# FFT filter and two MLPs on one core: half-height filter loads, a two-part store of the first spectrum, and an earlier first tile

## The chip, the core and the metric

The kernel is one program on one NeuronCore of a Trainium2 chip. Five engines run their own instruction streams and meet at semaphores: TensorE (PE, matmuls; its weight loads are shown as PEld), VectorE (DVE), ScalarE (ACT), GpSimd (POOL) and SyncE (SP), which here issues every DMA. The metric is the device time of one launch in microseconds (us). A median of 3 runs is taken; lower is better.

## The reference

```python
def _attn_ref(x, filt_r, filt_i):            # x: (2, 3008, 256)
    X = np.fft.rfft(x, axis=1)
    Y = X * (filt_r + 1j * filt_i)[None, :, :]
    return np.fft.irfft(Y, n=x.shape[1], axis=1)

def _moe_ref(x, w_gate, w_val, w_out, rms_g):   # 6016 tokens, 256 -> 1536 -> 256
    xn = x / np.sqrt(np.mean(x * x, axis=-1, keepdims=True) + 1e-06) * rms_g
    g = xn @ w_gate
    return ((g * (1.0 / (1.0 + np.exp(-g)))) * (xn @ w_val)) @ w_out

def _moe2_ref(x, w_in, w_out, s, b):            # 256 -> 2048 -> 256
    r = np.maximum(x @ w_in, 0.0)
    return (s * (r * r) + b) @ w_out
```

The three run one after the other, all in float32.

## The kernel before

**Front.** The FFT of length 3008 = 47 x 64 is done by matmuls in 16 chunks q (two batches of 8; a chunk is 32 of the 256 channels). For each chunk: DMA of a slab `x_ring` of 96 rows x 4 KB (`load_x`, ring of 3, so chunk q waits for `step1` of chunk q-3); PE `step1` (L341, the length-47 transform, two halves of 4 matmuls); ACT `u_out` (L533) copies it out; PE `step2` (L352, the length-64 transform); DVE `products` (L736 to L738, six multiplies with the filter, three for each half `dp`); POOL `total` (L913, adds the two product planes, one for each `dp`); PE `step3` (L362, inverse length 64); ACT `w_out_copy` (L539) writes the result into `w_fft[b]`. PE's order is software-pipelined: `step2(q)`, `step3(q-1, 0)`, both halves of `step1(q+1)`, `step3(q-1, 1)`.

The filter comes in 8 tiles `f_n` of 128 partitions x 6 KB (`load_f`); rows 64 to 127 are the same filter rows again. Its imaginary part is multiplied by a table of signs on POOL (`sign`, L906), +conj on the lower half and -conj on the upper one; `products(q)` of the first batch waits for sign q through `f_signed`. POOL does signs 0 and 1 first, and `sign(q+2)` behind the two totals of chunk q.

**Turning the layout.** When a batch's 8 chunks are done (`w_done` at 16, and at 32), two stores of 128 partitions x 12 j x 1 KB, 1.5 MB each, write `w_fft[b]` to a DRAM scratch `by_j`; tiles of 376 tokens are read back by `load_z` (two DMAs of 48 rows x 4 KB for one tile, ring of two, waiting for `step4` of the tile before last). PE `step4` (L373, inverse length 47, one call for each half of the channels) and DVE `copy_y` (L743) make the activations `y`. Of the first batch, tile 0 is worked into chunk 12: `step4(0, 0)` stands between `step2(12)` and `step3(11, 0)`, `step4(0, 1)` behind `step3(11, 1)`. The RMS norm of tile 0 (POOL `squares`, PE `sums` L384/L385, DVE, ACT `root`) follows in chunks 13 and 14.

**The two MLPs.** 16 tiles; in the first MLP each has 12 steps c of 12 + 6 matmuls (`gate_val`, `down`; every float32 product is three matmuls of a high and a low part), in the second 16 steps. While tile t runs, `step4(t+2, ...)` stands behind `down` of c = 5 and c = 7. Weights come from DRAM as float32 and are split into high and low parts by ACT, POOL and DVE between other work: `gate` and `down` during the front, `w_val` (`val_raw`) from chunk 14 on, `w_in2` (`in2_raw`) on POOL during the first MLP. `in2_raw` lies where filter tiles and `w_fft[1]` lay, so its load waits for the stores of batch 1 and the last products.

**SP's order** is the order of the DMA queue: x, tables and filters, with `gate` before x 4 and `down_raw` before x 6, then x 8 to 12, the stores of batch 0 between x 13 and x 14, tiles 0 and 1, `val_raw`, tiles 2 and 3 (each behind its `step4` wait), the stores of batch 1, `in2_raw`, and a loop for the other tiles.

Of the kernel before, what the change touches and what calls it, by code (L numbers as in the profile page):

```python
# [42 lines left out]
TB1, TB2, TB3, TB4 = 96, 120, 376, 504  # L43

# [22 lines left out]
def spectrum_tables():  # L67
# [21 lines left out]
    tab[:, TB1:TB2] = np.concatenate([conj, -conj])  # L89
# [6 lines left out]
def build(nc, by_j, x, filt, tab, step4, w_gate, w_val, w_out, rms_g, w_in2, w_out2, scale2, bias2, out):  # L96
    with ExitStack() as ctx:
# [140 lines left out]
        def _(sp):  # L238
# [90 lines left out]
        def _(pe):  # L329
# [197 lines left out]
        def _(a):  # L527
# [13 lines left out]

            def w1_high(i):
# [52 lines left out]
            w_out_copy(1, 1)  # L595
            for q in range(3, ALL - 1):
# [12 lines left out]
                w_out_copy(q - 1, 1)  # L609
                if 4 <= q < 4 + PIECES1D:  # L610
# [113 lines left out]
        def _(dve):  # L724
            nc.vector.memset(warm[:], 1.0).then_inc(warm_set, 1)
            def products(q, dp):

                dve.wait_ge(s2_mm, q + 1)
                if q < CHUNKS:
                    dve.wait_ge(f_signed, q + 1)  # L730
# [65 lines left out]
            for q in range(ALL):  # L796
                if q == 14:
# [5 lines left out]
                if q == 12:  # L803
                    copy_y(0, 0)
# [5 lines left out]
                if q == 12:  # L810
                    copy_y(0, 1)
# [84 lines left out]
        def _(gp):  # L896
# [118 lines left out]
```

## Time and profile before

| | |
|---|---|
| median of 3 runs | 1269.56 us (1268.67 to 1270.31) |
| the profiled execution | 1270.31 us, its span 1268.5 us |
| PE busy | 1248.8 us (98% of the span), 7268 matmuls |
| DVE, ACT, POOL busy | 685.4, 551.8, 163.7 us |
| mean granted clock of TensorE | 0.993 of full speed |
| DMA | 41.06 MB; 40.54 MB of them on SP's queue |

In slices of 1/40 of the span (31.7 us), the page shows PE at 8 8 8 9 tenths busy and 9 after that, the DMA engines at 9 6 7 3 2 tenths and near 0 later, and the granted clock below full speed in the first two slices. The MLPs fill the time from slice 4 on. A busy PE counts overlapping matmuls once.

### The profile page before, as it was taken

To read this page: it belongs to the slowest core of one execution; us is meant where nothing else is said; L and a number is where in the kernel's file an instruction comes from. 1 tells how busy PE (TensorE), PEld (TensorE's weight loads), DVE (VectorE), ACT (ScalarE), POOL (GpSimd) and SP (SyncE) were. 2 spreads that over 40 slices of the span, in tenths; PEclk is the share of its full clock that TensorE was granted. 3 is DMA by queue.
4 is the path that set the end of the run, shared out by engine and by line. 5 is a ranking of instruction groups with operands and counts; after the bars stand their busy time and mean duration, and the time that the engine had idled before them with its cause. 6 is when DMAs were issued, how large, how long until landed. Compare 5 with 4: busy or idle time off the path is not lost.

```text
span 1268.5 us, 20463 instructions
## 1 busy us (share of the span) xinstructions
PE 1248.8 (98%) x7268; PEld 1216.9 (96%) x7268; DVE 685.4 (54%) x1162; ACT 551.8 (44%) x1108; POOL 163.7 (13%) x165
## 2 busy tenths in 40 slices
PE   8889999999999999999999999999999999999998
PEld 5567999999999999999999999999999999999998
DVE  3566554545454355544554375555556556556555
ACT  2444434324334333433334365455445555455454
POOL 5665210111100111101120030000000000000000
PEclk8899999999999999999999999999999999999999
DMA  9673200000000000000010000000000000000000
GB/s 271 187 237 113 79 14 9 5 13 13 12 12 0 12 12 12 12 0 12 0 66 1 2 1 13 13 13 12 12 12 12 12 12 12 12 12 12 12 4 22
DMA packets 21239, 41.06 MB, mean 32 GB/s; under 512 B 2384, under 2 KB 16336, under 8 KB 20944
## 3 DMA queue, kind: packets, MB, share of 16 engines
q1 hardware_dynamic: 21200, 40.54, 10.5%
q8 instruction: 24, 0.39, 0.1%
q14 instruction: 15, 0.12, 0.0%
HBM read 28.08 MB, written 12.45 MB: 32 GB/s over the span
## 4 chain that ended last, share of the span: by engine, by line
PE 95%; DMA 2%; DVE 1%; POOL 0%; issue 0%; SPq 0%; ACT 0%; POOLq 0%; ACTq 0%
PE bank L388 30%; PE bank L389 30%; PE bank L390 29%; PE bank L373 2%; DMA x_ring<-x 2%; PE bank L341 2%; PE bank L362 1%; PE bank L352 1%; DMA z_ring<-by_j 0%; PE bank L384 0%; PE bank L385 0%; DVE rms L761 0%; DVE prod L738 0%; POOL spec L913 0%; DVE prod L737 0%
## 5 line engine op out<-in xcount | busy, mean ns | idle before, releaser
L783 DVE TENSOR_TENSOR h<-bank,act 128x376 f32<-128x376 f32 x192 | 104.6, 545 | 302.0 <-PE bank L390 293.5
L829 DVE SCALAR_TENSOR_TENSOR h<-act,sc 128x376 f32<-128x376 f32 x256 | 159.5, 623 | 189.6 <-ACT act L649 185.6
L562 ACT ACTIVATE act<-bank 128x376 f32<-128x376 f32 x192 | 92.9, 484 | 365.1 <-PE bank L390 364.9
L649 ACT ACTIVATE act<-bank 128x376 f32<-128x376 f32 x256 | 124.0, 484 | 223.9 <-PE bank L390 223.8
L389 PE MATMUL bank<-h_lo,out_hi 128*128 128x376 f32 x512 | 171.4, 335 | 0.0
L390 PE MATMUL bank<-h_hi,out_lo 128*128 128x376 f32 x512 | 171.4, 335 | 0.0
L388 PE MATMUL bank<-xn_hi,in_hi 128*128 128x376 f32 x512 | 171.1, 334 | 0.2 <-issue 0.2
L388 PE MATMUL bank<-h_hi,out_hi 128*128 128x376 f32 x512 | 171.2, 334 | 0.0
L389 PE MATMUL bank<-xn_lo,in_hi 128*128 128x376 f32 x512 | 171.1, 334 | 0.0
L390 PE MATMUL bank<-xn_hi,in_lo 128*128 128x376 f32 x512 | 170.4, 333 | 0.0
L835 DVE SCALAR_TENSOR_TENSOR h_lo<-h,bi,h_hi 128x376 fp32r<-128x376 f32 x256 | 157.6, 616 | 0.2 <-ACT h_hi L658 0.2
L658 ACT ACTIVATE h_hi<-h,bi 128x376 fp32r<-128x376 f32 x256 | 154.3, 603 | 1.9 <-DVE h L829 1.9
L388 PE MATMUL bank<-xn_hi,gate_hi 128*128 128x376 f32 x384 | 130.9, 341 | 1.2 <-DVE xn_lo L774 1.2
L389 PE MATMUL bank<-xn_lo,val_hi 128*128 128x376 f32 x384 | 128.8, 336 | 0.0
L390 PE MATMUL bank<-h_hi,down_lo 128*128 128x376 f32 x384 | 128.5, 335 | 0.0
L389 PE MATMUL bank<-h_lo,down_hi 128*128 128x376 f32 x384 | 128.5, 335 | 0.0
L388 PE MATMUL bank<-xn_hi,val_hi 128*128 128x376 f32 x384 | 128.3, 334 | 0.0
L389 PE MATMUL bank<-xn_lo,gate_hi 128*128 128x376 f32 x384 | 128.2, 334 | 0.0
L388 PE MATMUL bank<-h_hi,down_hi 128*128 128x376 f32 x384 | 128.2, 334 | 0.0
L390 PE MATMUL bank<-xn_hi,val_lo 128*128 128x376 f32 x384 | 128.2, 334 | 0.0
L390 PE MATMUL bank<-xn_hi,gate_lo 128*128 128x376 f32 x384 | 128.0, 333 | 0.0
L789 DVE TENSOR_TENSOR h_lo<-h,h_hi 128x376 fp32r<-128x376 f32 x192 | 116.7, 608 | 2.6 <-ACT h_hi L569 2.5
(81 smaller groups left out, 2057.2 us busy)
## 6 DMA issues: line engine op xcount, KB each, us to landing
x_ring<-x SPq DMA_DIRECT2D x16, 384.0 KB, 7.6
f<-filt SPq DMA_DIRECT2D x8, 768.0 KB, 14.5
by_j<-w_b SPq DMA_DIRECT2D x4, 1536.0 KB, 8.0
z_ring<-by_j SPq DMA_DIRECT2D x32, 192.0 KB, 2.9
out<-staged SPq DMA_DIRECT2D x32, 188.0 KB, 1.9
in_raw<-w_in SPq DMA_DIRECT2D x1, 2048.0 KB, 7.5
out_raw<-w_out SPq DMA_DIRECT2D x1, 2048.0 KB, 8.2
gate_raw<-w_gate SPq DMA_DIRECT2D x1, 1536.0 KB, 19.9
```

Source lines behind the costliest of these rows:

```text
L341: mm = nc.tensor.matmul(bank[g][:, i * XROWS:(i + 1) * XROWS], x_ring[:, q % XRING, g * GP + i], tabs[:, 0:TB1], start=True, stop=True)
L373: mm = nc.tensor.matmul(bank[7][:, k * BM:(k + 1) * BM], z_ring[:, par, k, half * P:(half + 1) * P], s4m[:], start=True, stop=True)
L388: nc.tensor.matmul(acc, hi, xh, start=first, stop=False)
L389: nc.tensor.matmul(acc, hi, xl, start=False, stop=False)
L390: return nc.tensor.matmul(acc, lo, xh, start=False, stop=final)
L562: nc.scalar.activation(act[:, c % 2], bank[2 * (c % 2)][:, 0:TILE], ACT.Silu).then_inc(silu_done, 1)
L649: nc.scalar.activation(act[:, c % 2], bank[c % 4][:, 0:TILE], ACT.Relu).then_inc(relu_done, 1)
L658: nc.scalar.activation(h_hi[:, c % 4], h[:, c % 2], ACT.Identity, bias=bi2[:]).then_inc(gh_done, 1)
L783: nc.vector.tensor_tensor(h[:, c % 2], bank[2 * (c % 2) + 1][:, 0:TILE], act[:, c % 2], ALU.mult).then_inc(hmul_done, 1)
L789: nc.vector.tensor_tensor(h_lo[:, c % 4], h[:, c % 2], h_hi[:, c % 4].bitcast(F32), ALU.subtract).then_inc(hl_done, 1)
L829: nc.vector.scalar_tensor_tensor(out=h[:, c % 2], in0=act[:, c % 2], scalar=sc2[:], in1=act[:, c % 2], op0=ALU.mult, op1=ALU.mult).then_in ...
L835: nc.vector.scalar_tensor_tensor(out=h_lo[:, c % 4], in0=h[:, c % 2], scalar=bi2[:], in1=h_hi[:, c % 4].bitcast(F32), op0=ALU.add, op1=ALU ...
```

## The change

1. **Filter loads.** DRAM holds each filter tile once, 64 rows, and `load_f` fills partitions 0 to 63 alone (384 KB instead of 768 KB). POOL's `sign` works on those 64 partitions. ACT makes the upper half: `f_real` copies the real part, `f_imag` the signed imaginary part times -1, and `products` of the first batch waits for `f_full`. POOL does signs 0, 1 and 2 first, and `sign(q+3)` behind the totals of chunk q.
2. **Scratch layout and stores.** `by_j` has the real/imaginary half c outermost, then j, then the 128 rows r of both batches. Batch 0 is stored in four DMAs: rows 0 to 15 of each half first (`w_near`), and rows 16 to 63 of each half later (`w_stored[0]`). Batch 1 is stored in two DMAs of 64 partitions x 24 j x 1 KB.
3. **Tiles.** Tile 0 is loaded when the near stores have landed, tile 1 behind the first far store. Tiles 2 and 3 are loaded by the loop, behind `in2_raw`.
4. **Order in chunks 11 to 13.** See the rows below; `squares(0)` on POOL moves between the two totals of chunk 12.

```diff
+NEAR = 16
...
             def load_f(n):
-                sp.dma_start(f_tiles[n][:].rearrange("p k c -> p (k c)"), filt[n]).then_inc(f_in[n], 16)
-
-            def store_w(b, n):
-                part = slice(n * NJ // 2, (n + 1) * NJ // 2)
-                sp.dma_start(by_j[b, part].rearrange("j p d -> p j d"), w_fft[b][:, part]).then_inc(w_stored[b], 16)
-
-            def load_z(b, r0, par):
+                sp.dma_start(f_tiles[n][0:NR].rearrange("p k c -> p (k c)"), filt[n]).then_inc(f_in[n], 16)
+
+            def store_w(b, c, r0, r1, done):
+                sp.dma_start(by_j[c, :, b * NR + r0:b * NR + r1].rearrange("j r d -> r j d"),
+                             w_fft[b][c * NR + r0:c * NR + r1]).then_inc(done, 16)
+
+            def load_z(t, par):
                 for rp in range(2):
                     sp.dma_start(z_ring[rp * 48:(rp + 1) * 48, par],
-                                 by_j[b].rearrange("j (c r) d -> (j c) r d", c=2)[:, bass.ds(r0 + rp * R4, R4)]
+                                 by_j.rearrange("c j r d -> (c j) r d")[:, bass.ds(t * 8 + rp * R4, R4)]
                                  ).then_inc(z_in[par], 16)
...
             sp.wait_ge(w_done, 2 * CHUNKS)
-            store_w(0, 0)
+            for c in range(2):
+                store_w(0, c, 0, NEAR, w_near)
             load_x(13)
-            store_w(0, 1)
+            sp.wait_ge(w_near, 32)
+            load_z(0, 0)
+            store_w(0, 0, NEAR, NR, w_stored[0])
+            load_z(1, 1)
+            store_w(0, 1, NEAR, NR, w_stored[0])
             load_x(14)
             load_x(15)
             sp.wait_ge(w_stored[0], 32)
-            load_z(0, 0, 0)
-            load_z(0, 8, 1)
             sp.dma_start(val_raw[:], w_val.rearrange("(h p) f -> p h f", p=P)).then_inc(val_in, 16)
-            for t in range(2, 4):
-                sp.wait_ge(s4_mm, 2 * t - 2)
-                load_z(0, 8 * t, t % 2)
             sp.wait_ge(w_done, 4 * CHUNKS)
-            for n in range(2):
-                store_w(1, n)
+            for c in range(2):
+                store_w(1, c, 0, NR, w_stored[1])
             sp.wait_ge(w_stored[1], 32)
             sp.wait_ge(p_done, 6 * ALL)
             sp.dma_start(in2_raw[:].rearrange("p (h f) -> p h f", h=HALVES),
                          w_in2.rearrange("(h p) f -> p h f", p=P)).then_inc(in2_in, 16)
-            for b in range(BATCH):
-                first = b * TILES // 2
-                with sp.Fori(4 if b == 0 else first, first + TILES // 2 - 1, 2) as i:
-                    for par in range(2):
-                        sp.wait_ge(s4_mm, 2 * (i + par) - 2)
-                        load_z(b, (i + par - first) * 8, par)
+            with sp.Fori(0, TILES - 3, 2) as i:
+                for par in range(2):
+                    sp.wait_ge(s4_mm, 2 * (i + par) + 2)
+                    load_z(i + par + 2, par)
...
             for q in range(3, ALL - 1):
                 step2(q)
                 if q == 12:
-                    pe.wait_ge(consts_in, 64)
-                    step4(0, 0, 0)
+                    step4(0, 0, 1)
                 step3(q - 1, 0)
                 step1(q + 1, 0)
                 step1(q + 1, 1)
-                step3(q - 1, 1)
-                if q == 12:
-                    step4(0, 0, 1)
                 if q == 13:
                     sums(0)
+                step3(q - 1, 1)
+                if q == 11:
+                    pe.wait_ge(consts_in, 64)
+                    step4(0, 0, 0)
...
+            def f_real(n):
+                a.wait_ge(f_in[n], 16)
+                nc.scalar.copy(f_tiles[n][NR:P, 0], f_tiles[n][0:NR, 0])
+
+            def f_imag(n):
+                a.wait_ge(f_signed, n + 1)
+                nc.scalar.activation(f_tiles[n][NR:P, 1], f_tiles[n][0:NR, 1], ACT.Copy, scale=-1.0).then_inc(f_full, 1)
...
             for q in range(ALL):
+                if q == 12:
+                    copy_y(0, 0)
                 if q == 14:
                     dve.wait_ge(consts_in, 64)
                     variance(0)
@@ -801,14 +824,12 @@
                     normalise(0)
                 products(q, 0)
                 if q == 12:
-                    copy_y(0, 0)
+                    copy_y(0, 1)
                 if q == 13:
                     square_low()
                 if q == 14:
                     xn_low(0, 0)
                 products(q, 1)
-                if q == 12:
-                    copy_y(0, 1)
...
-            for n in range(2):
+            for n in range(3):
                 sign(n)
             for q in range(ALL):
                 total(q, 0)
+                if q == 12:
+                    squares(0)
                 total(q, 1)
-                if q + 2 < CHUNKS:
-                    sign(q + 2)
+                if q + 3 < CHUNKS:
+                    sign(q + 3)
                 elif 7 <= q < 11:
                     w1_low(2 * (q - 7))
                     w1_low(2 * (q - 7) + 1)
                 elif q == 12:
-                    squares(0)
                     square_sum(0)
...
-    by_j = nc.dram_tensor("by_j", (BATCH, NJ, 2 * NR, DIM), F32, kind="Internal").ap()
+    by_j = nc.dram_tensor("by_j", (2, NJ, BATCH * NR, DIM), F32, kind="Internal").ap()
```

In ACT's new stream, between the copies of `step1` and `step3`, two instructions of 64 x 768 stand for each filter tile (16 in all): `f_real(n)` and `f_imag(n)` of tiles 0 and 1 around the copies of chunk 1, of tile 2 behind the first `w_out_copy`, of tile 3 behind `w_out_copy(1, 1)`, and of tile q+1 behind `w_out_copy(q-1, 1)` of chunks 3 to 6.

On POOL, at the program's start, the signs (`f_50` to `f_57` are filter tiles 0 to 7) and totals stood before like this:

```order
L906 TENSOR_TENSOR f_50<-f_50,tabs 128x768
L906 TENSOR_TENSOR f_51<-f_51,tabs 128x768
L913 TENSOR_TENSOR spec<-prod 128x384 x2
L906 TENSOR_TENSOR f_52<-f_52,tabs 128x768
L913 TENSOR_TENSOR spec<-prod 128x384 x2
L906 TENSOR_TENSOR f_53<-f_53,tabs 128x768
L913 TENSOR_TENSOR spec<-prod 128x384 x2
L906 TENSOR_TENSOR f_54<-f_54,tabs 128x768
L913 TENSOR_TENSOR spec<-prod 128x384 x2
L906 TENSOR_TENSOR f_55<-f_55,tabs 128x768
L913 TENSOR_TENSOR spec<-prod 128x384 x2
L906 TENSOR_TENSOR f_56<-f_56,tabs 128x768
```

They stand now like this:

```order
L927 TENSOR_TENSOR f_50<-f_50,tabs 64x768
L927 TENSOR_TENSOR f_51<-f_51,tabs 64x768
L927 TENSOR_TENSOR f_52<-f_52,tabs 64x768
L934 TENSOR_TENSOR spec<-prod 128x384 x2
L927 TENSOR_TENSOR f_53<-f_53,tabs 64x768
L934 TENSOR_TENSOR spec<-prod 128x384 x2
L927 TENSOR_TENSOR f_54<-f_54,tabs 64x768
L934 TENSOR_TENSOR spec<-prod 128x384 x2
L927 TENSOR_TENSOR f_55<-f_55,tabs 64x768
L934 TENSOR_TENSOR spec<-prod 128x384 x2
L927 TENSOR_TENSOR f_56<-f_56,tabs 64x768
L934 TENSOR_TENSOR spec<-prod 128x384 x2
```

Each sign from the fourth on stands one pair of totals earlier: sign 6 (`f_56`) stood behind the totals of chunk 4, and stands now ahead of them. On PE, from `step3(10, 1)` on, the chunks 11 to 13 were before (s4m is `step4`, spec `step3`, u_ring `step2`, x_ring `step1`, ss `sums`):

```order
L362 MATMUL bank<-spec,tabs 128x384
L352 MATMUL bank<-u_ring,tabs 128x384 x4
L373 MATMUL bank<-s4m,z_ring 128x96 x4
L362 MATMUL bank<-spec,tabs 128x384
L341 MATMUL bank<-tabs,x_ring 128x96 x8
L362 MATMUL bank<-spec,tabs 128x384
L373 MATMUL bank<-s4m,z_ring 128x96 x4
L352 MATMUL bank<-u_ring,tabs 128x384 x4
L362 MATMUL bank<-spec,tabs 128x384
L341 MATMUL bank<-tabs,x_ring 128x96 x8
L362 MATMUL bank<-spec,tabs 128x384
L384 MATMUL bank<-ss_hi,ones_r 128x376
```

They are now:

```order
L361 MATMUL bank<-spec,tabs 128x384
L372 MATMUL bank<-s4m,z_ring 128x96 x4
L351 MATMUL bank<-u_ring,tabs 128x384 x4
L372 MATMUL bank<-s4m,z_ring 128x96 x4
L361 MATMUL bank<-spec,tabs 128x384
L340 MATMUL bank<-tabs,x_ring 128x96 x8
L361 MATMUL bank<-spec,tabs 128x384
L351 MATMUL bank<-u_ring,tabs 128x384 x4
L361 MATMUL bank<-spec,tabs 128x384
L340 MATMUL bank<-tabs,x_ring 128x96 x8
L383 MATMUL bank<-ss_hi,ones_r 128x376
L384 MATMUL bank<-ss_lo,ones_r 128x376
```

Both halves of `step4` of tile 0 moved ahead, one to each side of `step2(12)`, and `sums(0)` moved ahead of `step3(12, 1)`. On SP, from the first store of batch 0 on (`w_b_59` is `w_fft[0]`, `w_b_60` is `w_fft[1]`), the queue was before:

```order
L250 DMA by_j<-w_b_59 128x12x256 [waits w_done]
L243 DMA x_ring<-x 96x1024 [waits s1_mm]
L250 DMA by_j<-w_b_59 128x12x256
L243 DMA x_ring<-x 96x1024 [waits s1_mm] x2
L254 DMA z_ring<-by_j 48x1024 [waits w_stored0]
L254 DMA z_ring<-by_j 48x1024 x3
L295 DMA val_raw<-w_val 128x2x1536
L254 DMA z_ring<-by_j 48x1024 [waits s4_mm]
L254 DMA z_ring<-by_j 48x1024
L254 DMA z_ring<-by_j 48x1024 [waits s4_mm]
L254 DMA z_ring<-by_j 48x1024
L250 DMA by_j<-w_b_60 128x12x256 [waits w_done]
```

It is now, from the second near store on:

```order
L250 DMA by_j<-w_b_59 16x24x256
L244 DMA x_ring<-x 96x1024 [waits s1_mm]
L255 DMA z_ring<-by_j 48x1024 [waits w_near]
L255 DMA z_ring<-by_j 48x1024
L250 DMA by_j<-w_b_59 48x24x256
L255 DMA z_ring<-by_j 48x1024 x2
L250 DMA by_j<-w_b_59 48x24x256
L244 DMA x_ring<-x 96x1024 [waits s1_mm] x2
L299 DMA val_raw<-w_val 128x2x1536 [waits w_stored0]
L250 DMA by_j<-w_b_60 64x24x256 [waits w_done]
L250 DMA by_j<-w_b_60 64x24x256
L305 DMA in_raw<-w_in 128x2x2048 [waits p_done,w_stored1]
```

Tile 0's loads no longer stand behind x 15, tile 1's stand between the far stores, and the four loads of tiles 2 and 3 that stood ahead of the batch-1 stores have gone behind `in_raw`.

## Rows read from the trace of the kernel before

**Rows 1.** Windows: start:end, each engine's busy time (instructions), PEclk, DMA share, GB/s.
```profile
0.00:120.00 120.00, 103.88 (x545) 72.98 (x546) 69.10 (x121) 49.17 (x103) 72.06 (x67) 0.93 0.68 199
...
120.00:1268.00 1148.00, 1144.87 (x6725) 1143.88 (x6724) 616.31 (x1042) 502.65 (x1005) 91.65 (x99) 1.00 0.05 15
```

**Rows 2.** Timeline of PE: start, duration, instruction, idle before and its releaser.
```profile
10.99 3.73 PE L341 MATMUL bank<-tabs,x_ring 128*128 128x96 f32 x16 [3.10 <-DMA x_ring<-x]
...
35.89 0.91 PE L362 MATMUL bank<-spec,tabs 128*128 128x384 f32 x2 [1.34 <-POOL spec L913]
...
40.66 0.91 PE L362 MATMUL bank<-spec,tabs 128*128 128x384 f32 x2
...
44.76 3.73 PE L341 MATMUL bank<-tabs,x_ring 128*128 128x96 f32 x16 [3.19 <-DMA x_ring<-x]
...
84.02 1.10 PE L373 MATMUL bank<-s4m,z_ring 96*128 96x96 f32 x8 [3.34 <-DMA z_ring<-by_j]
```

**Rows 3.** Chain that ended last: start, duration, what; x6 arrival, steady chunk, chunk 12.
```profile
52.08 0.84 PE bank L362 x2
...
57.69 1.76 PE bank L341 x16
...
61.61 0.84 PE bank L362 x2
...
76.75 1.77 PE bank L341 x16
...
85.97 3.21 PE bank L341 x16
```

**Rows 4.** Windows: the stretch behind the 44.76 us restart.
```profile
44.60:51.30 6.70, 6.54 (x24) 4.87 (x26) 0.26 (x1) 1.84 (x4) 3.51 (x3) 0.50 0.84 188
```

**Rows 5.** Chain: the two slab loads PE waited for, issue and time to landing.
```profile
2.14 8.81 DMA x_ring<-x
...
27.57 17.14 DMA x_ring<-x
```

**Rows 6.** Timeline of POOL: sign of filter tile 6 and the totals behind it.
```profile
47.79 1.81 POOL L906 TENSOR_TENSOR f<-f,tabs 128x768 f32<-128x768 f32 x1 [7.25 <-DMA f<-filt]
...
49.55 1.95 POOL L913 TENSOR_TENSOR spec<-prod 128x384 f32<-128x384 f32 x2
```

**Rows 7.** Timeline of ACT: a copy in chunk 7, and a two-tile cast.
```profile
67.26 0.48 ACT L539 COPY w_b<-bank 128x384 f32<-128x384 f32 x1 [0.62 <-PE bank L362]
...
102.06 0.82 ACT L580 CAST xn_hi<-y 128x752 fp32r<-128x752 f32 x1 [1.32 <-DVE y L768]
```

**Rows 8.** Windows: one slab load, one tile load, the batch-1 stores.
```profile
61.00:61.25 0.25, 0.25 (x4) 0.00 (x0) 0.00 (x0) 0.25 (x2) 0.25 (x1) 1.00 0.96 393
...
111.25:111.50 0.25, 0.25 (x3) 0.25 (x3) 0.00 (x0) 0.25 (x1) 0.25 (x2) 1.00 0.87 279
...
116.00:124.00 8.00, 8.00 (x48) 8.00 (x48) 4.11 (x7) 2.57 (x7) 6.44 (x6) 1.00 1.04 342
```

**Rows 9.** Timeline of SP: first store, batch-1 stores, `w_in2` load.
```profile
65.43 0.41 SPq L250 DMA_DIRECT2D by_j<-w_b  x1
...
114.83 1.52 SPq L250 DMA_DIRECT2D by_j<-w_b  x2
...
126.95 0.38 SPq L304 DMA_DIRECT2D in_raw<-w_in  x1
```

**Rows 10.** DMA issues in a window: count, KB each, us to landing; store 0, tile pair.
```profile
by_j<-w_b SPq DMA_DIRECT2D x1, 1536.0 KB, 7.0
...
z_ring<-by_j SPq DMA_DIRECT2D x2, 192.0 KB, 2.9
```

**Rows 11.** Timeline of POOL: first use of `w_in2`.
```profile
134.53 0.47 POOL L974 CAST in_hi<-in_raw 128x256 fp32r<-128x256 f32 x1 [11.80 <-DMA in_raw<-w_in]
```

**Rows 12.** Chain: `step4` of tile 2.
```profile
133.28 0.75 PE bank L373 x7
```

More of the change, by code:

```diff
@@ L76, in spectrum_tables @@
     step1 = np.zeros((HALVES, NM + 1, HALVES, 2, NJ))
-    step4 = np.zeros((2, NJ, 2, 2, NM + 1))
+    step4 = np.zeros((2, 2, NJ, 2, NM + 1))
     weight = np.where(j == 0, 1.0, 2.0)[:, None] / SEQ
@@ L80, in spectrum_tables @@
         step1[h, :NM, h, 0], step1[h, :NM, h, 1] = c47, -s47
-        step4[h, :, 0, h, :NM], step4[h, :, 1, h, :NM] = weight * c47.T, -weight * s47.T
+        step4[h, 0, :, h, :NM], step4[h, 1, :, h, :NM] = weight * c47.T, -weight * s47.T
     step2 = np.stack([np.concatenate([c64, -s64], axis=1), np.concatenate([s64, c64], axis=1)], axis=1)
@@ L88, in spectrum_tables @@
     tab[:XROWS, :TB1] = step1.reshape(XROWS, XROWS)
-    tab[:, TB1:TB2] = np.concatenate([conj, -conj])
+    tab[:NR, TB1:TB2] = conj
     tab[:, TB2:TB3] = np.concatenate([step2, step2]).reshape(P, -1)
@@ L170, in build @@
         f_in = [sem(f"f_in{n}") for n in range(CHUNKS)]
-        f_signed = sem("f_signed")
+        f_signed, f_full = sem("f_signed"), sem("f_full")
         s1_mm, u_done, s2_mm, p_done, spec_done = (sem(n) for n in ("s1_mm", "u_done", "s2_mm", "p_done", "spec_done"))
         s3_mm, w_done = sem("s3_mm"), sem("w_done")
-        w_stored = [sem("w_stored0"), sem("w_stored1")]
+        w_near, w_stored = sem("w_near"), [sem("w_stored0"), sem("w_stored1")]
         z_in = [sem("z_in0"), sem("z_in1")]
@@ L585, in square_high @@
                 nc.scalar.copy(ss_hi[:], sq[:, 0]).then_inc(ssh_done, 1)
-            for q in range(3):
-                u_out(q, 0)
-                u_out(q, 1)
+            u_out(0, 0)
+            u_out(0, 1)
+            f_real(0)
+            u_out(1, 0)
+            u_out(1, 1)
+            f_imag(0)
+            f_real(1)
+            f_imag(1)
+            u_out(2, 0)
+            u_out(2, 1)
             w_out_copy(0, 0)
+            f_real(2)
+            f_imag(2)
             w_out_copy(0, 1)
@@ L595, in _ @@
             w_out_copy(1, 1)
+            f_real(3)
+            f_imag(3)
             for q in range(3, ALL - 1):
@@ L609, in _ @@
                 w_out_copy(q - 1, 1)
+                if q + 1 < CHUNKS:
+                    f_real(q + 1)
+                    f_imag(q + 1)
                 if 4 <= q < 4 + PIECES1D:
@@ L729, in products @@
                 if q < CHUNKS:
-                    dve.wait_ge(f_signed, q + 1)
+                    dve.wait_ge(f_full, q + 1)
                 if q:
@@ L904, in sign @@
                 gp.wait_ge(f_in[n], 16)
-                fi = f_tiles[n][:, 1].rearrange("p (i j) -> p i j", j=NJ)
-                nc.gpsimd.tensor_tensor(fi, fi, tabs[:, TB1:TB2].unsqueeze(1).to_broadcast([P, 2 * PAIRS * HALVES, NJ]),
+                fi = f_tiles[n][0:NR, 1].rearrange("p (i j) -> p i j", j=NJ)
+                nc.gpsimd.tensor_tensor(fi, fi, tabs[0:NR, TB1:TB2].unsqueeze(1).to_broadcast([NR, 2 * PAIRS * HALVES, NJ]),
                                         ALU.mult).then_inc(f_signed, 1)
@@ L998 @@
     xs[:, :, :, :NM] = by_mr.transpose(0, 4, 3, 1, 6, 5, 2)
-    filt = np.stack([filt_r[rows], filt_i[rows]]).reshape(2, NR, NJ, HALVES, CHUNKS, 2, PAIRS).transpose(4, 1, 0, 5, 6, 3, 2).reshape(CHUNKS, NR, 4 * COLS)
-    arrays = {"x": xs.reshape(ALL, XROWS, PAIRS * P), "filt": np.concatenate([filt, filt], axis=1), "tab": tab,
+    filt = np.stack([filt_r[rows], filt_i[rows]]).reshape(2, NR, NJ, HALVES, CHUNKS, 2, PAIRS).transpose(4, 1, 0, 5, 6, 3, 2)
+    arrays = {"x": xs.reshape(ALL, XROWS, PAIRS * P), "filt": filt.reshape(CHUNKS, NR, 4 * COLS), "tab": tab,
               "step4": step4, "w_gate": moe_w_gate, "w_val": moe_w_val, "w_out": moe_w_out, "rms_g": moe_rms_g,
```

## The prediction

> **What bounds the kernel now.** I read three views. The windows come first [rows 1]: from 120 us to the end PE is busy for 1144.87 of 1148 us at the full clock, so nothing of the MLPs is to be had except by a new wait. In the first 120 us PE is busy for 103.88, so 16.1 us are idle, and part of the busy time is at half clock. PE's own timeline says what ended the idle time [rows 2]: slabs of x at 10.99 and 44.76 us (3.10 and 3.19 us of waiting), tile 0 from the scratch at 84.02 (3.34 us), and POOL's total at 35.89 (1.34 us). The chain of waits tells what a restart costs [rows 3]: from `step1` to the second `step3` behind it takes 61.61 - 57.69 = 3.92 us in a steady chunk, and 52.08 - 44.76 = 7.32 us behind the wait at 44.76, 3.4 us more. There the granted clock was 0.50, the 1.2 GHz level [rows 4]. The clock fell behind the waits of 3.10, 3.19 and 3.34 us, not behind the one of 1.34 us.
>
> So the front bounds what this change can reach, and in it the DMA queue up to some 45 us, and PE's own work (one chunk is 3.92 + 0.85 = 4.77 us) after it.
>
> **Part 1, half filters.** The queue is full up to 45 us. Slab 1 landed at 2.14 + 8.81 = 10.95 us and slab 6 at 27.57 + 17.14 = 44.71 [rows 5]. Between them lie 9024 KB (table 192, f 1 to 5 at 768, four slabs before slab 6 and itself at 384, gate and down at 1536), which is 9.24 MB in 33.8 us, 274 GB/s. A half filter, 384 KB, is worth 1.44 us at that rate.
>
> The saving does not arrive as slabs. POOL now does sign 6 ahead of the totals of chunk 4. Sign 6 started when f 6 had landed, at 47.79, and takes 1.81 us; one of the two totals behind it takes 0.98 [rows 6]. Seven halves (f 0 to f 6) fewer put f 6 at 47.79 - 10.1 = 37.7 us, sign 6 ends at 39.5, and the total at 40.5. `step3(4, 0)`, which ran at 40.66 [rows 2], waits for it, and `step1(6)` follows 0.7 us later at 41.2, against 44.76: a gain of 3.5 us. Slab 6 has landed by then (44.7 - 8.6 = 36.1 us). What is gained before that (slab 1 some 1.4 us earlier, the 1.34 us wait at 35.89 gone with the late sign of f 4) is inside this number: PE reaches `step3(4, 0)` at 40.66 - 1.44 - 1.34 = 37.9 and waits 2.6 us. That is nearer to the 3.10 us behind which the clock fell than to 1.34, so I take it that it falls again and its 3.4 us are paid as before. If f 6 is late by 1 us, the gain is 1 us less.
>
> Bounds: a half can save as much as its bytes at the best rate of the same slab form, or nothing. At 393 GB/s [rows 8] it would save 1.0 us if the other half stays at 1.88; by the mean rate it is 1.44; with no saving at all f 6 lands at 47.8, and the total ends at 50.6 instead of 40.5, `step1(6)` at 51.3, 6.5 us later than before. The break-even is f 6 at 41.3. I take 1.44, since the engines were busy all through with packets that each carry their bytes.
>
> ACT gets 16 instructions. The trace has none of 64 x 768; the nearest is a cast of 128 x 752, 0.82 us [rows 7], so 1.66 us a chunk. In chunks 3 to 5 ACT has that. In chunk 6 it also splits `gate`, and it sat idle for only 0.62 us ahead of the next copy at 67.26 [rows 7]: 1.0 us too much, partly behind `step1`'s 1.76 us. I take 0.6 us lost over the two chunks behind it; the bounds are 0 and 2 x 1.0. POOL's sign on 64 instead of 128 partitions costs the same per element of a row; I take 1.81 again.
>
> **Part 2, tile 0 earlier.** From `step1(12)` at 76.75 to `step1(13)` at 85.97 are 9.22 us [rows 3]; 4.77 is the steady chunk and 0.86 half of `step4`, so 3.6 were lost, and 3.21 - 1.76 = 1.45 more to the clock. If tile 0 is on time, 5.0 us are gained. It is: the first store was issued at 65.43 [rows 9], and took 7.0 us to landing [rows 10] for 1.57 MB, which at 342 GB/s [rows 8] is 4.6 us of data and 2.4 of latency. Two near stores of 0.79 MB together are 2.3 + 2.4 + 0.4 of issue, 70.5; the tile's pair needs 2.9 us [rows 10] and an issue or two, 74 us. `step4(0, 0)` wants it at 79.1, so 5 us are to spare. Queued behind it are two far stores, tile 1 and slab 14: 3.5 MB, 10.3 us at 342 GB/s, so slab 14 lands at about 82. PE wants it at 79.1 + 0.86 + 1.5 + 0.86 + 0.7 + 1.8 + 0.7 + 1.5 + 0.7 = 87.7. That is free too, with 5.6 us to spare. `w_val` follows in time for chunk 14. `sums(0)` and the squares a step earlier take some of the wait for the norm's chain; I take 0.5 us (bounds -0.5 and 1.2).
>
> **Part 3, tile 2 later.** This is the new wait. The stores of batch 1 were issued at 114.83 and `w_in2` at 126.95, when they had landed [rows 9]; POOL used it at 134.53 [rows 11]. Tile 2 was long there and `step4(2, 0)` ran at 133.28 [rows 12]. Now tile 2 stands in the queue behind 2 MB of `w_in2`: it cannot land before 134.5 + 1.4 us (its 393 KB at 279 GB/s [rows 8]) = 135.9. PE waits 2.7 us, in a place where all it lost before was nothing, with all the down products queued behind it. Both ends of this shift together with the front, so the earlier gain does not help. The clock falls probably; at chunk 12 that cost 1.45. Sum 4.2. Bounds: 1.5 (the two transfers overlap, the clock stays) to 6.1 (3.4 for the clock).
>
> **The sum.** 3.5 - 0.6 + 5.0 + 0.5 - 4.2 = 4.2 us less. Against the profiled execution's own 1270.31 that is 1266.1, and since that run lies 0.75 above the median of the runs shown, 1265.4.
>
> **Transfers of few partitions.** A load of a 96-row slab reached 393 GB/s in a quarter of a microsecond, and the pair of 48-row tile loads, whose first one lies wholly in rows 0 to 47, 279 GB/s [rows 8]. Filters now fill rows 0 to 63 alone, and the stores read 16, 48 or 64 rows.
>
> The Trainium skill ("SBUF — State Buffer", the section on the DMA port swizzle) says that partitions 0 to 63 reach no more than half of the ports, and gives 196 GB/s for 64 rows against 328 for 128, which is 0.6. This trace shows 279 for 48 rows, above its figure, and nothing for 64 rows or for stores. By its ratio, put into the working of the first rival below, the sum would be some 11 us slower, 1281.
>
> **Rivals.**
> 1. Slower: transfers of a part of the partitions move at 279 / 393 = 0.71 of the rate [rows 8]. For it speaks that pair of rows itself, the same bytes in two loads of 48 rows; against it that two loads have two starts, and that all 16 engines were busy either way. A half then saves 1 - 0.5 / 0.71 = 30% of 2.88, 0.85 us; f 6 lands at 41.8, and `step1(6)` is 0.5 us later than before instead of 3.5 earlier. Slab 14 comes 5.1 us later, still in time. The batch-1 stores (3.15 MB, 9.2 us) take 3.8 more, so tile 2 costs 8.0. Sum: -0.5 + 5.0 - 0.6 + 0.5 - 8.0 = 3.6 slower, 1273. It decides from a rate of 0.82 down: there the seven halves and the two stores together have lost the 4.2. Chance 0.2 for all that is slower.
> 2. The clock stays up behind the waits for sign 6 and for tile 2, since both are under 3.10 us: 3.4 + 1.45 more, 1260.6. It speaks for it that the front's other waits are gone. Chance 0.22.
> 3. The gain is eaten: f 6 lands 2 to 3 us late (the filters' rate is not the mean) and tile 2 costs its 6.1: 1269, no change. Chance 0.14.
> My forecast has 0.44.
>
> **Range and chances.** The forecast's own range is 1262.5 to 1268. With rival 2 and a little of better filters the low end is 1258.5; the high end 1274 takes in rival 1 and leaves out what is worse, some 0.1. What a measurement tells from no change is 0.2%, 2.5 us. Faster: the forecast nearly whole and rival 2, 0.66; same: 0.14; slower: 0.20.
>
> **What would show it.** In the new profile: POOL's sign 6 at 37.7 and `step3(4, 0)` at 40.6 with POOL as releaser after 2.6 us; no wait of `step1(6)`; whether the clock is 0.50 behind it; `step4(0, 0)` near 75 to 76 with no DMA wait; no wait for slab 14; `step4(2, 0)` waiting 2.7 us for `z_ring`, behind `w_in2`. I am wrong if f 6 lands after 41, if slab 14 is waited for, or if the batch-1 stores take over 14 us. A `step4(2, 0)` that waits for nothing would put the time at or under 1262.

## The result and the profile after

The changed kernel takes 1281.01 us (median of 4 runs, 1279.98 to 1282.63), the kernel before 1269.12 us beside it (4 runs); the ratio is 1.0094, 95% interval 1.0078 to 1.0109. It is slower by 0.9%. The forecast was 1265.4 us in a range up to 1274: direction and range are both wrong. The profiled execution took 1282.06 us (span 1280.1), 11.75 more than the one of before.

The windows of the changed kernel's first 120 us and of the rest answer to [rows 1]; the two under them are the first pair of stores and the pair of batch 1. Columns: us, then busy time (instructions) of PE, PEld, DVE, ACT and POOL, granted clock, DMA share, GB/s.

```profile
63.00:72.00 9.00, 9.00 (x58) 5.90 (x54) 7.30 (x14) 5.83 (x14) 8.33 (x8) 1.00 0.80 166
...
116.00:132.00 16.00, 16.00 (x94) 16.00 (x93) 7.60 (x14) 7.26 (x16) 6.75 (x6) 1.00 0.87 197
...
0.00:120.00 120.00, 104.01 (x539) 71.63 (x540) 68.40 (x120) 61.61 (x119) 71.84 (x66) 0.90 0.63 159
120.00:1279.00 1159.00, 1148.03 (x6731) 1146.71 (x6729) 616.42 (x1042) 503.05 (x1006) 92.74 (x100) 1.00 0.05 16
```

The rest of the program, where PE was idle for 3 us, now has 11 us without work. The stores of batch 1, the same 3.15 MB as before, move at 197 GB/s where [rows 8] had 342. In the window of the first pair everything together moves at 166 GB/s, which is 1.49 MB in 9 us; the pair itself is 0.79 MB of that, and the rest is slab loads. In the batch-1 window the DMA engines count as busy for 0.87 of the time: a high share does not mean that they move much.

PE's timeline shows where it waits, in rows that answer to [rows 2] (start, duration, instruction, idle time before it and its releaser).

```profile
8.36 2.02 PE L340 MATMUL bank<-tabs,x_ring 128*128 128x96 f32 x16 [0.48 <-DMA x_ring<-x]
17.60 1.65 PE L361 MATMUL bank<-spec,tabs 128*128 128x384 f32 x2 [2.37 <-POOL spec L934]
...
41.80 1.65 PE L361 MATMUL bank<-spec,tabs 128*128 128x384 f32 x2 [3.12 <-POOL spec L934]
...
76.63 1.03 PE L372 MATMUL bank<-s4m,z_ring 96*128 96x96 f32 x8
...
92.18 3.73 PE L340 MATMUL bank<-tabs,x_ring 128*128 128x96 f32 x16 [6.53 <-DMA x_ring<-x]
109.21 0.88 PE L361 MATMUL bank<-spec,tabs 128*128 128x384 f32 x2 [0.66 <-ACT w_b L538]
...
142.68 2.02 PE L372 MATMUL bank<-s4m,z_ring 96*128 96x96 f32 x8 [8.44 <-DMA z_ring<-by_j]
151.82 1.03 PE L372 MATMUL bank<-s4m,z_ring 96*128 96x96 f32 x8
```

Tile 0 is on time (76.63, no wait). Slab 14 is waited for at 92.18 for 6.53 us, and tile 2 at 142.68 for 8.44 us. The same places in the kernel before, from its own timeline:

```profile
92.90 1.92 PE L341 MATMUL bank<-tabs,x_ring 128*128 128x96 f32 x16
...
104.62 0.44 PE L388 MATMUL bank<-xn_hi,gate_hi 128*128 128x376 f32 x1 [1.16 <-DVE xn_lo L774]
...
108.26 0.88 PE L362 MATMUL bank<-spec,tabs 128*128 128x384 f32 x2 [0.66 <-ACT w_b L539]
...
133.12 1.03 PE L373 MATMUL bank<-s4m,z_ring 96*128 96x96 f32 x8
...
140.22 1.03 PE L373 MATMUL bank<-s4m,z_ring 96*128 96x96 f32 x8
```

Reading one against the other gives the account. PE was ready for slab 14 at 92.18 - 6.53 = 85.65, 7.25 us ahead of before: the front did gain. The wait takes 6.53 of that back (0.72 ahead at `step1(14)`). Up to 109.21, where the kernel is 0.95 behind 108.26, it loses another 1.67. That is a net figure: from `step1(14)` to the next `step4` it takes 12.51 us instead of 9.43, 3.1 us of clock, and 1.4 us come back, because the wait of 1.16 us ahead of the first MLP matmul (104.62 before) is gone. From there to `step4(2, 1)` the kernel falls to 151.82 - 140.22 = 11.6 us behind: 8.44 of waiting and 2.2 of clock. That is the whole difference of the two profiles.

The granted clock behind the three longest waits, in windows, answers to [rows 4]:

```profile
41.10:47.90 6.80, 6.10 (x20) 4.59 (x20) 3.90 (x7) 1.43 (x3) 5.70 (x5) 0.50 0.12 27
88.90:99.10 10.20, 6.92 (x24) 5.39 (x26) 0.82 (x2) 1.87 (x5) 0.99 (x1) 0.50 0.55 200
136.70:146.90 10.20, 4.22 (x16) 4.22 (x17) 0.55 (x1) 0.23 (x1) 1.12 (x2) 0.50 0.63 201
```

The waits of 6.53 and 8.44 us each have a half-clock stretch of 10.2 us, the wait of 3.12 one of 6.8. Parts of these stretches lie inside the waits; what costs is PE's work in them.

The chain of waits says what held the two transfers up (start, duration, what):

```profile
63.04 0.35 SPq L250
...
63.43 8.48 DMA by_j<-w_b
...
74.41 3.52 SPq L255
...
77.97 2.49 SPq L250
...
80.51 11.63 DMA x_ring<-x
...
92.18 3.73 PE bank L340 x16
...
115.78 0.71 SPq L250
...
116.53 16.32 DMA by_j<-w_b
...
132.87 0.40 SPq L305
...
134.22 8.42 DMA z_ring<-by_j
...
142.68 2.02 PE bank L372 x8
```

Every link is the stores. The near pair lands at 71.91, 8.9 us after 63.04. Behind the first far one SP itself stands for 3.52 and 2.49 us over single issues, so slab 14 goes out at 80.51 and then needs 11.63 us. The batch-1 pair needs 17.1 us from 115.78 to the issue of `w_in2` at 132.87; before it was 12.1 [rows 9].

### The profile page after: what moved, and what is told of

Its sections match the earlier page's. It is cut to its first block, busy times and chain, and to the rows that moved or that the text cites. A ratio compares the mean times of both kernels' runs of the same rounds, so it can differ in the third digit from the quotient of the medians.

```text
span 1280.1 us, 20492 instructions
## 1 busy us (share of the span) xinstructions
PE 1252.0 (98%) x7268; PEld 1218.3 (95%) x7268; DVE 684.8 (53%) x1162; ACT 564.7 (44%) x1124; POOL 164.6 (13%) x165
## 4 chain that ended last, share of the span: by engine, by line
PE 93%; DMA 4%; SPq 1%; issue 1%; POOL 0%; ACT 0%; DVE 0%; POOLq 0%
PE bank L387 29%; PE bank L388 29%; PE bank L389 29%; PE bank L372 2%; DMA by_j<-w_b 2%; PE bank L361 2%; PE bank L340 1%; PE bank L351 1%; DMA x_ring<-x 1%; DMA f<-filt 1%; DMA z_ring<-by_j 1%; SPq L255 0%; SPq L250 0%; POOL spec L934 0%; ACT w_b L538 0%
## 6 DMA issues: line engine op xcount, KB each, us to landing
f<-filt SPq DMA_DIRECT2D x8, 384.0 KB, 10.9
```

## The experiments

They came in the order in which the questions did. "Before" and "changed" are the two kernels.

**1. Is it tile 2's place?** Changed, with tiles 2 and 3 read ahead of the batch-1 stores again:

```diff
+            for t in range(2, 4):
+                sp.wait_ge(s4_mm, 2 * t - 2)
+                load_z(t, t % 2)
             sp.wait_ge(w_done, 4 * CHUNKS)
...
-            with sp.Fori(0, TILES - 3, 2) as i:
+            with sp.Fori(2, TILES - 3, 2) as i:
```

> The changed kernel with the loads of tiles 2 and 3 put back ahead of the batch-1 stores; nothing else. Theory 'late tile': in the changed kernel PE waited 8.44 us for tile 2 at 142.68 us and then ran at half clock, 11.6 us lost from there to step4 of the second half (133.28 to 140.38 us before, 142.68 to 151.98 now, of which 0.95 is older). Without it the time is 1281.0 - 10.6 = 1270.4. Rival 'slow stores alone': if the slow batch-1 stores hurt in another way (w_in2 arrives late for POOL), the time stays above 1275.

Measured 1274.01 us (10 runs), ratio 1.0032 [1.0017, 1.0047]. PE's timeline has `step4(2, 0)` without a wait, and slab 14 waited for as before the edit:

```profile
44.15 1.65 PE L364 MATMUL bank<-spec,tabs 128*128 128x384 f32 x2 [3.63 <-POOL spec L937]
93.07 3.73 PE L343 MATMUL bank<-tabs,x_ring 128*128 128x96 f32 x16 [6.45 <-DMA x_ring<-x]
...
134.55 1.03 PE L375 MATMUL bank<-s4m,z_ring 96*128 96x96 f32 x8
```

By the medians 7.0 us of the 11.9 hang on tile 2. The two profiled executions are 10.2 us apart (spans 1280.1 and 1269.9), close to the 10.65 us that the changed kernel's profile puts at tile 2, but the profiled execution of this run was one of its fastest (1271.85 us, where the ten runs go from 1271.37 to 1277.19). So tile 2's price is 7 to 10 us, and these runs do not tell it closer. Slab 14 keeps its wait.

**2 and 3. Which part costs?** Filters alone on the kernel before (half tiles, POOL's signs one chunk earlier, ACT's copies), and the rest of the change without them:

```diff
-                sp.dma_start(f_tiles[n][:].rearrange("p k c -> p (k c)"), filt[n]).then_inc(f_in[n], 16)
+                sp.dma_start(f_tiles[n][0:NR].rearrange("p k c -> p (k c)"), filt[n]).then_inc(f_in[n], 16)
...
-                if q + 2 < CHUNKS:
-                    sign(q + 2)
+                if q + 3 < CHUNKS:
+                    sign(q + 3)
```

> The kernel before with the half-height filters, ACT's copies and the new places of the signs alone; scratch layout, stores, tiles and order as before. At the last w_out_copy of batch 0 the changed kernel was 2.4 us ahead (63.04 against 65.43). If that lead is kept to the end: 1269.1 - 2.4 = 1266.7. Rival: the lead is lost again at tile 0 or in ACT's stream in chunks 14 and 15, and the time is within 0.5 us of before.

> The changed kernel with full-height filters loaded as before and the signs in their old places; new scratch layout, stores, tiles and order. If the two parts add: 1281.0 + 2.4 = 1283.4. If the loss comes from the filters' side at all, it is below 1275.

Filters alone: 1269.77 us (12 runs), ratio 0.9998 [0.9984, 1.0013]. Stores and order alone: 1282.12 (4 runs), ratio 1.0089 [1.0059, 1.0118], with slab 14 waited for 6.04 us and tile 2 for 8.97:

```profile
93.88 3.73 PE L340 MATMUL bank<-tabs,x_ring 128*128 128x96 f32 x16 [6.04 <-DMA x_ring<-x]
...
144.65 2.02 PE L372 MATMUL bank<-s4m,z_ring 96*128 96x96 f32 x8 [8.97 <-DMA z_ring<-by_j]
```

The whole loss is in the stores and their order; the filters bring nothing. PE's timeline of the filters-only kernel:

```profile
42.33 1.65 PE L362 MATMUL bank<-spec,tabs 128*128 128x384 f32 x2 [4.86 <-POOL spec L935]
81.90 2.00 PE L373 MATMUL bank<-s4m,z_ring 96*128 96x96 f32 x8 [3.85 <-DMA z_ring<-by_j]
```

Slab 6 is no longer waited for; `step3(4, 0)` stands 4.86 us behind POOL's total in its place.

**4. Rows or number of rows?** A program of DMAs alone, each group issued when the last has landed: pairs of stores out of a tile of 128 rows x 24 j x 256 in the layouts of the kernels, and groups of four filter loads. `wide` stores 12 j of all 128 rows; `part` stores 24 j of as many rows as its last number says, from the row before it on; `go` waits. The six pairs of stores are: 128 rows; rows 0 to 63 twice; rows 32 to 95 twice; rows 0 to 63, then 64 to 127; the near pair; the far pair.

```diff
+                wide(0, 0, 12)
+                wide(0, 12, 12)
+                go()
+                part(0, 0, 0, 64)
+                part(1, 0, 0, 64)
+                go()
+                part(0, 0, 32, 64)
+                part(1, 0, 32, 64)
+                go()
+                part(0, 0, 0, 64)
+                part(0, 64, 64, 64)
+                go()
+                part(0, 0, 0, 16)
+                part(0, 64, 64, 16)
+                go()
+                part(0, 16, 16, 48)
+                part(0, 80, 80, 48)
+                go()
```

> Only DMAs, none of the reference: pairs of stores of 1 KB pieces to a DRAM scratch, waited for pair by pair, then groups of four filter-like loads, all twice. Theory 'queue order': 64 rows x 24 KB move as fast as 128 rows x 12 KB, 3.15 MB in 9.2 + 2.4 = 11.6 us. Theory 'partitions': rows 0 to 63 take 3.15 MB / 197 GB/s + 1.5 = 17 us, as the batch-1 stores did. Within that, if the reason is which rows (the half of the ports that rows 0 to 63 reach), rows 32 to 95 are as fast as 128 rows, 11.6; if it is the number of rows, they take 17 too; one store from rows 0 to 63 and one from 64 to 127 take 17 if the two run one behind the other, 11.6 if they share. Near pair (2 x 16 rows, 0.79 MB): 4.7 by queue order, 8 to 9 by partitions. Four loads of 128 rows x 6 KB (3.15 MB): about 9.5; four of 64 rows (1.57 MB): 5.5 by queue order, 9 by partitions.

The windows lie inside the six pairs of stores, then inside four loads of 128 rows, of rows 0 to 63, and of rows 32 to 95; the last two numbers of a line are the DMA share and GB/s.

```profile
7.50:17.50 10.00, 0.00 (x0) 0.00 (x0) 1.00 0.95 315
18.50:34.50 16.00, 0.00 (x0) 0.00 (x0) 1.00 0.88 196
35.50:45.50 10.00, 0.00 (x0) 0.00 (x0) 1.00 0.94 314
46.50:62.50 16.00, 0.00 (x0) 0.00 (x0) 1.00 0.88 196
63.50:71.50 8.00, 0.00 (x0) 0.00 (x0) 1.00 0.73 98
72.00:86.50 14.50, 0.00 (x0) 0.00 (x0) 1.00 0.75 161
88.00:97.00 9.00, 0.00 (x0) 0.00 (x0) 1.00 0.90 350
98.00:107.00 9.00, 0.00 (x0) 0.00 (x0) 1.00 0.80 175
108.00:114.50 6.50, 0.00 (x0) 0.00 (x0) 1.00 0.72 242
```

The same 3.15 MB takes 10.6 us from 128 rows, 17.2 from rows 0 to 63, and 10.9 from rows 32 to 95. So at 64 rows it is not the number of rows and not the order of the addresses in DRAM (24 j x 64 rows both times): it is which rows. Two stores of opposite halves behind each other (17.0 us) gain nothing over two of the same half. That pair is what the changed kernel issues for batch 1. The two pairs of batch 0 fare worse: the near pair, 16 rows each, takes 8.7 us for 0.79 MB, the far pair, 48 rows each, 15.6 us for 2.36 MB, together 24.3 us for the bytes that the full-height pair moves in 10.6. Four loads of rows 0 to 63 took 9.9 us, almost as long as four of 128 rows with twice the bytes (10.3); four of rows 32 to 95 took 7.6. It is one launch, in which every group ran twice; the second pass repeats the stores within 0.1 us and the loads within 0.5.

The Trainium skill ("SBUF — State Buffer", the section on the DMA port swizzle) has partitions 0 to 63 on one half of the ports, and bit 6 of the partition's number choosing the half; it gives 196 GB/s and 328. The trace agrees, with 196 and 315, and rows 32 to 95, which have bit 6 in both states, move at 314. The same page of the Trainium skill, in its section on issuing two DMAs to hit both halves, says that they serialize; the 17.0 us agree.

**5. Is slab 14 the other half?** Experiment 1, with tile 1 and slab 14 ahead of the far stores:

```diff
-            store_w(0, 0, NEAR, NR, w_stored[0])
             load_z(1, 1)
-            store_w(0, 1, NEAR, NR, w_stored[0])
             load_x(14)
+            store_w(0, 0, NEAR, NR, w_stored[0])
             load_x(15)
+            store_w(0, 1, NEAR, NR, w_stored[0])
```

> e1 (tiles 2 and 3 early) with tile 1 and slab 14 ahead of both far stores and slab 15 between them. Theory 'queue place': PE's 6.45 us wait for slab 14 and the half clock behind it (4 us) were paid for the place behind 2.3 MB of slow stores; both go, 1270 to 1272 becomes 1262 to 1264. Rival 'the wait moves': w_val must wait for the far stores, which end no earlier than before (about 91 us), lands at about 99 to 100, and ACT needs it in chunk 14 some 8 us before that; since ACT copies step1's result behind it, PE waits there and the time stays within 3 us of e1.

Measured 1269.04 us (9 runs; a tenth took 2742.61 us, for a reason that nothing here shows, and is left out), ratio 1.0007 [0.9992, 1.0022]: 0.25% better than experiment 1, and just level with before. Slab 14 is on time, and the wait has moved. First PE's row, then ACT's, of this kernel:

```profile
94.38 1.62 PE L364 MATMUL bank<-spec,tabs 128*128 128x384 f32 x2 [6.56 <-ACT w_b L541]
```

```profile
92.93 0.92 ACT L559 CAST val_hi<-val_raw 128x384 fp32r<-128x384 f32 x2 [7.74 <-DMA val_raw<-w_val]
```

`w_val` waits for the far stores; ACT waits for `w_val` in its own stream, and the copy that PE needs is queued behind that. The traffic is the same, so something is late wherever it stands.

**6. Another way to an early tile 0.** Before, with its two full-height stores of batch 0 back to back and tile 0 read ahead of slab 15:

```diff
             store_w(0, 0)
-            load_x(13)
             store_w(0, 1)
+            load_x(13)
             load_x(14)
-            load_x(15)
             sp.wait_ge(w_stored[0], 32)
             load_z(0, 0, 0)
+            load_x(15)
             load_z(0, 8, 1)
```

> The kernel before with both full-height stores of batch 0 issued one behind the other at w_done, then slabs 13 and 14, then tile 0 ahead of slab 15; layout, filters and PE's order as before. Both stores move 3.15 MB at 342 GB/s and land at 65.4 + 0.4 + 9.2 + 2.4 = 77.4 instead of 78.5, and tile 0's load no longer stands behind slab 15's wait for step1(12); it lands at about 80.8 and PE wants it at 80.6. Of the 3.34 us wait some 3 go, and the 1.45 us of half clock: 4.4 less, 1265.3. Rival: slab 13, now behind both stores, lands after 81.5 and PE waits for it instead: no gain.

Measured 1267.81 us (12 runs), ratio 0.9985 [0.9973, 0.9998]: barely a gain, less than half of the 4.4 us expected. The stores landed as expected, 11.8 us after the first issue. Tile 0's pair then took 5.7 us, behind slabs 13 and 14 in the queue, where [rows 10] has 2.9, so that the wait at tile 0 only went from 3.34 [rows 2] to 2.44 us.

**7. Was it POOL's order?** Experiment 2 with one edit: the signs in the places they had before, behind the totals of chunk q - 2.

```diff
-            for n in range(3):
+            for n in range(2):
                 sign(n)
...
-                if q + 3 < CHUNKS:
-                    sign(q + 3)
+                if q + 2 < CHUNKS:
+                    sign(q + 2)
```

> e2 (half filters alone) with POOL's signs in their old places, two ahead at the start and sign q+2 behind the totals of chunk q. Theory 'sign 6 blocks': in e2 sign 6 waited 7.01 us for f 6 ahead of the totals of chunk 4, and PE 4.86 us behind them, with half clock for 6.8 us after. With the old places the totals of chunk 4 do not wait; sign 6 is needed for products 6 only, and PE waits for slab 6 or not at all: step1(6) at 38 to 39 us instead of 43.9, 4 to 8 us less than e2 up to there, and 1262 to 1265 at the end. Rival: the wait moves to products 5 or 6 (ACT's copy of the filter stands in the way of u_out), and the time is within 1 us of e2.

Measured 1263.68 us (12 runs), ratio 0.9957 [0.9942, 0.9971]: a clear gain. PE's rows, then POOL's sign 6:

```profile
34.31 0.91 PE L362 MATMUL bank<-spec,tabs 128*128 128x384 f32 x2
38.27 2.15 PE L341 MATMUL bank<-tabs,x_ring 128*128 128x96 f32 x16 [3.04 <-DMA x_ring<-x]
...
76.52 1.10 PE L373 MATMUL bank<-s4m,z_ring 96*128 96x96 f32 x8 [3.72 <-DMA z_ring<-by_j]
```

```profile
40.64 1.80 POOL L928 TENSOR_TENSOR f<-f,tabs 64x768 f32<-64x768 f32 x1 [5.74 <-DMA f<-filt]
```

`step3(4, 0)` runs at 34.31 and not at 42.33 as in experiment 2, and `step1(6)` at 38.27, where it ran at 43.77 in experiment 2 and at 44.76 before. That is one execution against one, and this front moves by some us from execution to execution: with full-height filters `step1(6)` runs at 44.76, 44.88, 41.24 and 42.67 (before, experiments 3, 6 and 8), with half filters and the old signs at 38.27, 41.36 and 38.28 (experiments 7, 9 and 10). The means are 4.1 us apart, 0.7 us for each of the six halves ahead of slab 6. Sign 6 comes no earlier than in experiment 2 (39.53 there), but behind it nobody is waiting yet. Tile 0 runs 7.5 us earlier than before [rows 2], which is the difference of the two spans (1261.0 against 1268.5).

**8. What does the order alone cost?** Before, with full-height stores, tiles 2 and 3 behind `w_in2`:

```diff
-            for t in range(2, 4):
-                sp.wait_ge(s4_mm, 2 * t - 2)
-                load_z(0, 8 * t, t % 2)
             sp.wait_ge(w_done, 4 * CHUNKS)
...
                          w_in2.rearrange("(h p) f -> p h f", p=P)).then_inc(in2_in, 16)
+            for t in range(2, 4):
+                sp.wait_ge(s4_mm, 2 * t - 2)
+                load_z(0, 8 * t, t % 2)
```

> The kernel before with the loads of tiles 2 and 3 moved behind w_in2's load, all stores full-height. This is the step of the prediction by itself: tile 2 lands at about 135.9 to 136.5, PE wants it at 133.1 and waits 2.7 to 3.4 us; with the clock falling once, 4.2 to 5 us more, 1274. If order alone explains the 8.44 us wait of the changed kernel, PE waits over 7 us here too and the time is 1280.

Measured 1275.5 us (4 runs), ratio 1.0055 [1.0034, 1.0077], 5.7 us by the medians. The chain of waits:

```profile
112.17 0.40 SPq L250
112.61 11.66 DMA by_j<-w_b
124.29 0.38 SPq L301
...
125.22 8.85 DMA z_ring<-by_j
134.12 2.02 PE bank L373 x8
```

```profile
144.34 1.03 PE L373 MATMUL bank<-s4m,z_ring 96*128 96x96 f32 x8
```

PE waited 3.50 us for tile 2, and from `step4(2, 0)` to `step4(2, 1)` (the second row, from PE's timeline) took 144.34 - 134.12 = 10.2 us instead of 140.22 - 133.12 = 7.1, so 3.1 us of clock. The forecast had 2.7 of wait and 1.45 of clock. With the half-row stores the same chain is 17.1 us from store to `w_in2` instead of 12.1, and the wait 8.44 instead of 3.50: the 5 us between are the store rate.

**9. Does the early sign cost the changed kernel too?** Changed, with the edit of experiment 7:

> The changed kernel with POOL's signs back in their old places (sign q+2 behind the totals of chunk q); all else as changed. If the early signs take the filters' gain in the changed kernel too, its front is some 4 to 6 us earlier up to chunk 12, but slab 14 then waits behind the same stores: if those begin earlier with the front, all moves together and the time is 1275 to 1277 us; sign 6 then ends nothing and step1(6) is released by x_ring near 38 us. Rival: the queue behind the stores sets the end whatever the front does, and the time stays at 1281.

Measured 1276.70 us (6 runs), ratio 1.0060 [1.0040, 1.0080], against 1.0094 with the early signs. The kernel moves by 4 us as expected, and all the rest stays: slab 14 waited for 6.18 us at 90.16, tile 2 for 8.90 at 139.95.

**10. The best version.** Experiment 7 with the store order of experiment 6:

> The kernel before with half-height filters, POOL's signs in their old places, and both full-height stores of batch 0 issued back to back, tile 0 read ahead of slab 15. If the two gains are independent (half filters 6.1 us, stores together 1.9 us), 1261.8 us, ratio about 0.9942. Rival: the front is now limited by PE's own work and by tile 0 alone, so the wait at tile 0 is as long as with the filters alone (3.7 us) and the time stays at 1263.7.

Measured 1263.06 us (9 runs), ratio 0.9952 [0.9935, 0.9969]. The wait at tile 0 shrank to 2.24 us, but the time cannot be told from experiment 7's: both beat the kernel before by 0.4 to 0.5% and the changed one by 1.4%. In the profiled execution `step1(6)` had the same wait as in experiment 7, and another clock behind it:

```profile
38.28 3.73 PE L341 MATMUL bank<-tabs,x_ring 128*128 128x96 f32 x16 [3.04 <-DMA x_ring<-x]
```

## Why the prediction was wrong

**The step that failed** is the rate of the stores. The prediction took 342 GB/s, the rate of 128-row stores [rows 8], for stores of 16, 48 and 64 rows. Three terms hang on it:

- "Two near stores ... 70.5" needed 5.1 us and took 8.9. Tile 0 had enough slack for that, and its term was right: from `step1(12)` to being ready for `step1(14)` the changed kernel is 4.9 us shorter, where 5.0 were forecast.
- "Slab 14 lands at about 82 ... free too, with 5.6 us to spare": it landed at 92.14. PE wanted it at 85.65 (the forecast said 87.7), waited 6.53 us and lost 1.67 net behind it. A term of 0 was 8.2 us.
- Tile 2, costed at 4.2 us, cost 10.65 (8.44 + 2.2) in the profile. Experiment 8 has the term at full-rate stores: 5.7 us, inside its bounds of 1.5 to 6.1, and the sentence "the earlier gain does not help" held.

With the 2.4 us that the front had gained at `step1(12)` this is 2.4 + 4.9 - 8.2 - 10.65 = -11.6 us, the difference of the two profiles.

**The evidence for that rate was there, and was weighed wrongly.** The first rival was the right mechanism with too mild a price: it read 0.71 from two windows of a quarter of a microsecond [rows 8], where stretches of 10 and 16 us give 196 / 315 = 0.62. The 279 GB/s row was put down as "48 rows", but the second load of that pair fills rows 48 to 95, which lie on both sides of row 64; experiment 4 has loads on both sides of row 64 at 242 GB/s where rows 0 to 63 have 175. It was no sample of rows 0 to 63. The rival also let slab 14 through as "still in time", at one rate for all row counts. Alone, the near and the far pair take 13.7 us more than the full-height pair (24.3 against 10.6), far more than the 5.6 us to spare; in the kernel slab 14 came 10.1 us after the forecast.

With the ratio of 0.6 that the Trainium skill ("SBUF — State Buffer", the section on the DMA port swizzle) gives, the prediction has a sum of 1281. Redone at 0.6, the first rival's own terms give 8.6 us slower, 1278: `step1(6)` 3.2 us later and tile 2 at 10.3. The 2.7 us up to 1281 are what slab 14 would add (6.9 us later on 5.6 to spare, and 1.45 of clock), which is not written down. That 1281 is the measured time to the microsecond is partly luck: its filters cost 3.2 us where the changed kernel's front gained 2.4, and its slab 14 has 2.7 where 8.2 were lost.

**Filters.** Forecast: f 6 at 37.7, `step1(6)` 3.5 us earlier. In this pair of profiles f 6 is at 39.00 and `step1(6)` at 43.24, 1.5 us earlier, and a half was worth 8.79 / 7 = 1.26 us, not 1.44. Over all executions even this gain is not to be seen: with the early signs `step1(6)` runs at 43.24, 45.59, 43.77 and 40.75 (changed, experiments 1, 2 and 5), on average as late as with full-height filters (43.3 against 43.4), and experiment 2's time says the same. The order of POOL was read rightly and its price as well, but it was treated as a given of part 1 and never priced as a part of its own: by the medians of experiments 2 and 7 the early sign costs 6.1 us (5.2 by their ratios), all that the half filters give. ACT's copies, a term of 0.6, show no wait in chunks 6 to 8.

**The clock.** The fall behind the wait for sign 6 was forecast and came, behind 3.12 us of waiting and not 2.6. Rival 2, no fall behind a wait under 3.10 us, is out: the changed kernel fell already behind its wait of 2.37 us, where `step3` at 17.60 takes 1.65 us and not 0.91. But the length of a wait alone does not say whether the clock falls. In experiment 1 a wait of 2.28 us at the same place has 0.91 behind it, and ahead of `step1(6)` the same 3.04 us had 2.15 us of `step1` behind it in experiment 7 and 3.73 in experiment 10. Nor does a longer wait cost more: 3.1 us of clock behind 3.50 us (experiment 8), 3.1 behind 6.53, some 2 behind 8.44. The forecast's 1.45 for tile 2 was too little for either.

What is open: alone, four half loads were almost as slow as four whole ones, and in the kernel each half saved about 0.7 us with the old signs. There full-height transfers stand between them. Whether these use the idle half meanwhile was not separated. A version whose stores or filters lie in rows 32 to 95 was not tried in the kernel, only by itself. The rates behind the near and far stores inside the kernel were not separated either; they come from the program of DMAs alone.

## What to carry to other kernels

Price a DMA by the rows that it touches, not by its bytes: before halving a tile's height, ask on which rows the half lies, and sum the whole queue behind it at the lower rate. Splitting a 128-row store into an upper and a lower half moves the first tile forward and everything queued later back; the slack of the last transfer decides. A wait on an in-order engine belongs behind the work that others already wait for: one sign placed a chunk too early cost as much as halving every filter load had won.

## What the runs showed that I had not expected

- A pair of stores of 64 rows is as fast as one of 128 if it straddles row 64: 10.9 us for 3.15 MB from rows 32 to 95, against 10.6, and 17.2 from rows 0 to 63. For loads the gain is smaller: 7.6 us against 9.9 for 1.57 MB.
- Narrower stores are slower still for their bytes: 98 GB/s from 16 rows and 161 from 48, where 64 rows of one half have 196.
- The issuing engine can be held up while much is queued: SP stood 3.52 and 2.49 us over single issues behind the far stores, so a slow store also delays the issue of what is behind it. It is not peculiar to half-height stores: in the kernel before, slab 6's issue at 27.57 took 6.24 us.
- Waits of 6.5 and 8.4 us each had 10.2 us at half clock, where the wait of 3.12 had 6.8, but the long waits themselves cover 3.3 and 6.0 us of theirs.
